# First batch: where the weights' low parts, the range tests and the row flips stand in the order of work

## What is computed

```
attention: state = alpha[t] * state + k[t] (x) v[t];  y[t] = q[t] . state      (alpha in 0.8 to 1.0)
stage 1:   u  = x + Re(FFT over channels (FFT over tokens (x)))
           un = (u - mean) / sqrt(var + 1e-6)
           x2 = u + relu(un @ w_ch1) @ w_ch2          (w_ch1 384x1536, w_ch2 1536x384)
stage 2:   h  = relu(x2^T @ w_tok1) @ w_tok2          (768x256, 256x768)
           u2 = x2 + h^T
           out = u2 + relu(u2 @ w2_ch1) @ w2_ch2
```

## Time and profile before

| what | us |
|---|---|
| median of three runs | 924.83 |
| the profiled execution's own time | 926.65 |
| its span, first to last instruction | 924.9 |
| PE busy | 894.7 (97%) |
| DVE busy | 469.0 (51%) |
| ACT busy | 311.9 (34%) |
| POOL busy | 207.0 (22%) |
| mean granted TensorE clock | 0.990 of full |

### The profile page before, as it was taken

The page is one execution under the profiler, slowest core; times in us unless marked ns, Lnnn a source line. Parts: engine busy times, 40 slices in busy tenths (PEclk is TensorE's granted clock), DMA queues, the critical chain, the costliest instruction groups (busy, mean ns, idle before and its releaser), DMA issues.

```text
span 924.9 us, 14637 instructions
## 1 busy us (share of the span) xinstructions
PE 894.7 (97%) x5376; PEld 861.2 (93%) x5376; DVE 469.0 (51%) x1127; ACT 311.9 (34%) x826; POOL 207.0 (22%) x360
## 2 busy tenths in 40 slices
PE   8978899999999998999999999999999999999998
PEld 5767799998999998999999998999999999999998
DVE  6777876648867658766472216321332142323121
ACT  4663455332555325553323233211121112112111
POOL 3784333302333112333012332000200020002000
PEclk9799999999999999999999999999999999999999
DMA  9803122003030040220017002100200020000000
GB/s 273 323 1 86 31 59 58 27 19 99 26 103 14 27 116 27 59 59 27 1 70 231 26 1 83 46 26 1 76 1 26 0 77 0 26 0 26 0 26 26
DMA packets 14360, 50.81 MB, mean 55 GB/s; under 512 B 1408, under 2 KB 5632, under 8 KB 12368
## 3 DMA queue, kind: packets, MB, share of 16 engines
q1 hardware_dynamic: 13728, 46.95, 16.2%
q0 software_dynamic: 576, 3.15, 0.9%
HBM read 40.66 MB, written 9.44 MB: 54 GB/s over the span
## 4 chain that ended last, share of the span: by engine, by line
PE 87%; DVE 8%; ACT 2%; issue 1%; POOL 1%; DMA 0%; DVEq 0%; ACTq 0%; SPq 0%
PE bank L1141 24%; PE bank L1143 24%; PE bank L1142 24%; PE bank L1155 4%; PE bank L1174 3%; PE bank L1179 2%; PE bank L1164 1%; PE bank L1327 1%; DVE ext L721 1%; PE bank L1321 1%; PE bank L1149 1%; PE bank L1386 1%; PE bank L1274 1%; DVE suf L751 1%; DVE hl L1016 1%
## 5 line engine op out<-in xcount | busy, mean ns | idle before, releaser
L1016 DVE SCALAR_TENSOR_TENSOR hl<-bank,hh 128x384 fp32r<-128x384 f32 x192 | 106.9, 557 | 333.8 <-ACT hh L635 333.7
L635 ACT ACTIVATE hh<-bank 128x384 fp32r<-128x384 f32 x192 | 94.3, 491 | 357.8 <-PE bank L1143 357.8
L1141 PE MATMUL bank<-nh,w1h 128*128 128x384 f32 x288 | 102.6, 356 | 0.5 <-DVE nl L972 0.5
L1141 PE MATMUL bank<-w2h,hh 128*128 128x384 f32 x288 | 101.4, 352 | 0.2 <-DVE u L1031 0.2
L1141 PE MATMUL bank<-u2h,w3h 128*128 128x384 f32 x288 | 97.0, 337 | 0.9 <-DVE u2l L1097 0.9
L1143 PE MATMUL bank<-nh,w1l 128*128 128x384 f32 x288 | 97.5, 339 | 0.0
L1142 PE MATMUL bank<-nl,w1h 128*128 128x384 f32 x288 | 97.2, 337 | 0.0
L1143 PE MATMUL bank<-w2h,hl 128*128 128x384 f32 x288 | 97.0, 337 | 0.0
L1141 PE MATMUL bank<-w4h,hh 128*128 128x384 f32 x288 | 96.9, 337 | 0.0
L1142 PE MATMUL bank<-w2l,hh 128*128 128x384 f32 x288 | 96.6, 335 | 0.0
L1143 PE MATMUL bank<-u2h,w3l 128*128 128x384 f32 x288 | 96.3, 334 | 0.0
(11 more groups left out here) (145 smaller groups left out, 1896.5 us busy)
## 6 DMA issues: line engine op xcount, KB each, us to landing
qkap<-qka SPq DMA_DIRECT2D x15, 1008.0 KB, 6.4
vt<-v SPq DMA_DIRECT2D x16, 288.0 KB, 7.8
raw_a<-w_ch SPq DMA_DIRECT2D x6, 768.0 KB, 10.1
mid<-u SPq DMA_DIRECT2D x8, 576.0 KB, 3.0
raw_b<-w_ch SPq DMA_DIRECT2D x6, 768.0 KB, 5.8
xr<-mid SPq DMA_DIRECT2D x8, 576.0 KB, 4.3
out<-u SPq DMA_DIRECT2D x8, 576.0 KB, 2.8
raw_t<-w_tok SPq DMA_DIRECT2D x2, 768.0 KB, 6.3
```

The lines of the kernel that those rows point to most:

```text
L635: act.activation(hh[:, s % 4, :], bank[s % 2][:, 0:HALF], ACT.Relu).then_inc(s_hhi, 1)
L1016: dve.scalar_tensor_tensor(out=hl[:, s % 4, :], in0=bank[s % 2][:, 0:HALF], scalar=0.0, in1=hh[:, s % 4, :].bitcast(F32), op0=ALU.max, op1 ...
L1141: pe.matmul(out_ap, wh, rh, start=first, stop=False)
```

## The change

- `LOW_AT`, `LATE_LOW_AT`: four half pieces of the low parts are written in visits 12, 14, 16 and 18 of batch 0 (before: eight, in the odd visits from 9); four once the edge rows of batch 0 are copied (before: once x is split); the last four in visits 0, 2, 4 and 6 of batch 1, that is beside MLP 0. PE's wait for all twelve becomes three waits, at MLP steps 2, 6 and 10.
- `RANGE_AT`: the 8 reductions of batch 0 stand one each at the end of visits 1, 2, 5, 7, 9, 11, 13 and 15 (before: in visits 2 and 3, 8 and 9, 10 and 11, 14 and 15).
- `flipped`: the flips of batch 0 go to banks 2 to 4 in place of 5 to 7, `f1` of batch 0 does not wait for their copies, and ACT splits the first half of x before it copies the flips.
- `edge_rows` moves from slot 39 to slot 35, behind the third split of g.
- POOL's v terms of tile 2 wait until the normalised row tile 2 is written (`un_ready`), in every batch.
- `fourier_u` of tiles 4 and 5 moves from slot 45 to slot 46, behind `norm_split` of tile 2, in every batch.
- `fill` gives one spare matmul behind visit 22 and four behind visit 23 (before: none behind either).

```diff
--- before.py
+++ after.py
@@ -36,6 +36,10 @@
 PAUSES = (3, 7, 14, 21, 28)
 WARM = 8
 FILL = {31: 5, 42: 6, 44: 4, 45: 1, 46: 2}
+LOW_AT = (12, 14, 16, 18)
+LATE_LOW_AT = (0, 2, 4, 6)
+RANGE_AT = {1: (1, 0), 2: (1, 1), 5: (2, 0), 7: (2, 1), 9: (0, 0), 11: (3, 0), 13: (3, 1), 15: (0, 1)}
+RANGED = (0, 2, 4, 7)
 VISIT = dict(zip([h for h in range(31) if h not in PAUSES], range(-2, STEPS)))
 SUMS_AT = 31
 F1_AT = 33
@@ -289,6 +293,10 @@
     def turned(a, k):
 
         return visit_bank(a, k - 2)[:, T_AT:T_AT + PR]
+
+    def flipped(a, j):
+
+        return bank[(5 if a else 2) + j][:, 0:DM]
 
     def bad_sum(a):
 
@@ -483,27 +491,29 @@
                 pool.wait_ge(s_rows, a + 1)
                 for j in (1, 2):
                     pool.wait_ge(s_vc, a * 3 + j + 1)
+                    if j == 2:
+                        pool.wait_ge(*un_ready(a, 2))
                     for dst, src, w, op in v_terms(a, j):
                         pool.tensor_tensor(dst, src, w, op).then_inc(s_pv, 1)
 
             pool.wait_ge(s_qk0, 16)
             prep(0, 0)
             tables = ((dfth, dft[0]), (dftl, dft[1]), (csh, cs[0]), (csl, cs[1]))
-            wi = 0
             for k in range(-2, STEPS):
                 visit(0, k)
                 if 3 <= k < 7:
                     pool.dma_start(tables[k - 3][0][:], tables[k - 3][1].bitcast(F32R)).then_inc(s_table, 16)
-                elif k >= 9 and k % 2:
-                    weight_lo(wi)
-                    wi += 1
-            pool.wait_ge(s_xlo, 2 * KT)
-            for i in range(wi, 2 * NA):
+                elif k in LOW_AT:
+                    weight_lo(LOW_AT.index(k))
+            pool.wait_ge(s_rows, 1)
+            for i in range(len(LOW_AT), 2 * NA - len(LATE_LOW_AT)):
                 weight_lo(i)
             for a in range(B):
                 if a:
                     for k in range(-2, STEPS):
                         visit(a, k)
+                        if a == 1 and k in LATE_LOW_AT:
+                            weight_lo(2 * NA - len(LATE_LOW_AT) + LATE_LOW_AT.index(k))
                 fourier_v(a)
                 if a + 1 < B:
                     prep(a + 1, 0)
@@ -569,7 +579,7 @@
                     act.wait_ge(s_mid, MID_PRIMED + 32 * (a - 1))
                 for j in range(3):
                     act.wait_ge(s_flip, a * 3 + j + 1)
-                    act.activation(us[a % 2][:, 2 * j + 1, :], bank[5 + j][:, 0:DM], ACT.Copy).then_inc(s_flipc, 1)
+                    act.activation(us[a % 2][:, 2 * j + 1, :], flipped(a, j), ACT.Copy).then_inc(s_flipc, 1)
 
             def split_x(a, part):
                 act.wait_ge(s_fold, a * 7 + (4, 7)[part])
@@ -615,9 +625,13 @@
 
             def tail(a, h):
                 if h == SUMS_AT:
-                    copy_flipped(a)
-                if h in (SUMS_AT, SUMS_AT + 1):
-                    split_x(a, h - SUMS_AT)
+                    if a:
+                        copy_flipped(a)
+                    split_x(a, 0)
+                if h == SUMS_AT + 1:
+                    if a == 0:
+                        copy_flipped(a)
+                    split_x(a, 1)
                 if 0 <= h - F1_AT < 2 * KT:
                     split_g(a, h - F1_AT)
                 if h in V_AT:
@@ -761,7 +775,7 @@
                 buf, cols = chunk(a, k)
                 decay = buf[0:PR, 2, cols]
                 if k % NC == 0 and (a or k):
-                    dve.wait_ge(s_ext, a * (2 * NU) + 2 * ((k // NC + 1) if a else (3, 1, 2, 4)[k // NC]))
+                    dve.wait_ge(s_ext, a * (2 * NU) + (2 * (k // NC + 1) if a else RANGED[k // NC]))
                 dve.wait_ge(s_inv, a * STEPS + k + 1)
                 dve.tensor_tensor_scan(decay, decay, nothing(a).to_broadcast([PR, P]), inv[0:PR, j:j + 1],
                                        ALU.mult, ALU.add).then_inc(s_pre, 1)
@@ -840,14 +854,14 @@
                     range_flag(a)
                 if 0 <= k + 1 < STEPS:
                     attn_scores(a, k + 1)
-                if k % NC == 3 and 0 <= k and k // NC + 1 < NU:
+                if a and k % NC == 3 and 0 <= k and k // NC + 1 < NU:
                     extreme(a, k // NC + 1, 1)
                 attn_state(a, k + 1)
                 prep(a, k + 3)
-                if k % NC == 2 and k // NC + 1 < NU:
+                if a and k % NC == 2 and k // NC + 1 < NU:
                     extreme(a, k // NC + 1, 0)
-                if a == 0 and k in (10, 11):
-                    extreme(a, 0, k - 10)
+                if a == 0 and k in RANGE_AT:
+                    extreme(a, *RANGE_AT[k])
                 if k + 2 == FLAG:
                     range_test(a)
                 if k in (FLAG + 2, FLAG + 3):
@@ -977,10 +991,10 @@
                     fold(a)
                 if h in (SUMS_AT + 1, SUMS_AT + 2):
                     split_x(a, h - SUMS_AT - 1)
-                if h == F1_AT + 2 * KT:
-                    edge_rows(a)
                 if 0 <= h - F1_AT < 2 * KT:
                     split_g(a, h - F1_AT)
+                if h == F1_AT + 2:
+                    edge_rows(a)
                 if h == 40:
                     fourier_v(a)
                     for i in range(2):
@@ -1003,7 +1017,7 @@
                     norm_rows(a, 2)
                 for t in NORM_AT.get(h, ()):
                     norm_split(a, t)
-                if h == 45:
+                if h == 46:
                     for i in range(2):
                         fourier_u(a, 4, 2, i)
                 if h == SLOTS - 1 and a + 1 < B:
@@ -1215,14 +1229,13 @@
                 if a:
                     pe.wait_ge(s_nlo, a * NC)
                 for j in range(3):
-                    pe.matmul(bank[5 + j][:, 0:DM], flip[:, :], x[:, 5 - j, :], start=True, stop=True
-                              ).then_inc(s_flip, 1)
+                    pe.matmul(flipped(a, j), flip[:, :], x[:, 5 - j, :], start=True, stop=True).then_inc(s_flip, 1)
 
             def f1(a, i):
 
                 part, t = i // KT, i % KT
                 pe.wait_ge(s_xlo, a * 6 + i + 1)
-                if i == 0:
+                if i == 0 and a:
                     pe.wait_ge(s_flipc, a * 3 + 3)
                 if i >= 3:
                     pe.wait_ge(s_glo, a * (2 * KT) + i - 2)
@@ -1329,7 +1342,7 @@
 
             for k in range(-2, STEPS):
                 visit(0, k)
-                fill(1 if 0 <= k < STEPS - 2 else 0)
+                fill(0 if k < 0 else 4 if k == STEPS - 1 else 1)
             pe.wait_ge(s_const2, 32)
             pe.wait_ge(s_table, 64)
             for h in range(SUMS_AT, SLOTS):
@@ -1344,8 +1357,8 @@
                             pe.wait_ge(s_nlo, b * NC + 3 * (s // NF) + 3)
                         mlp_in(b, s, w1h, w1l, nh, nl).then_inc(s_hp, 1)
                     elif s >= 2:
-                        if b == 0 and s == 2:
-                            pe.wait_ge(s_wlo, 2 * NA)
+                        if b == 0 and s in (2, 6, 10):
+                            pe.wait_ge(s_wlo, 2 * (KT + 1 + (s - 2) // FG))
                         mlp_out(b, s - 2, w2h, w2l, s_x2, b * NC + X2_PRIMED)
                     elif b:
                         mlp_out(b - 1, MLP - 2 + s, w2h, w2l, s_x2, (b - 1) * NC + X2_PRIMED)
```

## The result

The changed kernel takes 929.19 us (median of 13 runs, 926.63 to 937.58), the kernel before on the same chip 924.86 (13 runs, 924.09 to 928.88): ratio 1.0049, 95% interval 1.0029 to 1.007. That is 4.3 us slower, and 3.9 above the forecast of 925.3, inside its range. The profiled execution took 932.0 us, with a span of 930.2.

The account below looks back on a forecast made before the run. PE bounds the kernel, busy 97% of the span, with most idle time in batch 0's first 108 us. Terms sum to +0.5 on the profiled 926.65, giving 927.15; less 1.8 for the median, 925.3 us, range 919.5 to 930.0.

Parts of the forecast that it names:

- the collision: After `f1` in batch 0, POOL's later pieces hold up DVE's four v additions, delaying PE: 3.7 us, plus 0.9 of half clock.
- the two losses: POOL's later pieces holding DVE's additions (3.7 us, 0.9 for half clock) and `fourier_u` delaying PE at batch ends (2.9).
- The second rival: Half clock stays in the visits, so the 3.0 us isn't gained: 929.6 us, chance 0.2.
- Clock in the visits: Batch 0's visits: evenly spaced reductions remove the half clock from 36.8 to 47.0 us; gain 3.0, bounds 0 and 5.1.
- the range test is free: In batch 0's visits, POOL's pieces no longer hold DVE's range test: 0.7 us gained.
- Low parts in the visits: Batch 0's visits: four POOL pieces instead of eight delay products less; gain 1.3 us, bounds 0 and 3.8.
- Range tests: Batch 0's visits: one pair of reductions and six single ones cost DVE 4.1 us, not 5.3; gain 1.2.
- Sums, flips, split: Batch 0 after the visits: undisturbed sums and full-clock flips let `f1` begin 5.6 us behind the sums, not 7.7; gain 2.1.
- spare matmuls: The one behind visit 22 delays visit 23's output, costing 0.3 us; four behind visit 23 fill PE's wait and keep clock.
- Four later pieces: Behind `f1` in batch 0, pieces waiting for edge rows delay DVE's additions and PE's second u product: 3.7 us lost.
- the half clock behind the stall: After PE idles 4.7 us in batch 0, spare matmuls run at half clock in half of executions: 0.9 us lost.
- `fourier_u`: At three batch ends, running it behind the last split makes PE wait longer: 2.9 us lost, bounds 0 and 3.1.

Follow-up runs that it names:

- a3: Changed kernel with POOL's four later pieces waiting for the split of x again and `fourier_u` of tiles 4 and 5 back in slot 45: 920.91 us, ratio 0.9933.
- a1: Changed kernel with one edit undone: POOL's four later pieces wait for the split of x again, not the edge rows; 924.72 us, ratio 0.9984.
- a2: Changed kernel with one edit undone: `fourier_u` of tiles 4 and 5 back in slot 45; 925.79 us, ratio 0.9998.
- a4: a3 with ACT's first high part of a weight in visit 8 instead of 6: 919.34 us, ratio 0.9926.
- c3: a4 without the line that holds back POOL's v terms of tile 2: 918.96 us, ratio 0.9933.
- b3: Kernel before with only the new places of the range reductions, at most one a visit: 921.52 us, ratio 0.9961.
- a6: a4 with POOL's four pieces in visits 10, 12, 14 and 18 instead of 12, 14, 16 and 18: 918.32 us, ratio 0.9924.
- b1: Kernel before with only `fourier_u` of tiles 4 and 5 moved to slot 46: 929.24 us, ratio 1.0046.
- c1: Kernel before with only the changed tail of batch 0 (flips' banks, `f1` without a wait, ACT's split first, spare matmuls): 925.59 us, ratio 0.9997.
- c2: Kernel before with only the low parts' new places and PE's three waits, four pieces still waiting for the split of x: 923.15 us, ratio 0.9976.
- b2: Kernel before with only the edge rows copied earlier, behind the split of g, and POOL's four later pieces waiting for them: 931.99 us, ratio 1.0069.

## Why the prediction was right, and where it failed

**The number** was 3.9 us low. The mechanism that I called likeliest (gains in the visits and before `f1`, eaten by the collision and the batch ends) is there in all its pieces. By the times, the two losses were sized too small: 10.7 us between after and a3, where my terms have 7.5. The gains were about right: without the losses my terms leave 7.0, and a3 is 6.2 under the kernel before (4.5 to 7.8). 3.2 and 0.8 make up the 3.9 but for a tenth. The second rival, the half clock that stays in the visits, comes to 929.6 by its working, next to the measured 929.19, but that is luck: by it a3 would be 7.5 lower, 922.1 and 2.7 under the kernel before, which is outside a3's interval.

**Clock in the visits (-3.0).** In the profiles of after's own code this gain isn't there: 10.2 and 3.4 us of half clock in after, 6.8 in a1, 3.4 in a2, 10.2 in a3, 6.8 in a4, none in c3, against 10.2 in before. The cause that I had named, the pairs of reductions, is borne out by the thirteen profiles, and with the range tests alone (b3) the visits kept 1.00 and the time fell by 3.6 us. What I had wrong is that nothing would take the place of the pairs. In after it was two stops of PE, 2.10 for `qz` behind ACT's late weight load and 1.70 for the flag; in the other kernels with after's visits it was the second alone. So the step that failed is the sentence that the range test is free, in the next term. How the times of a3 hold most of the gain all the same isn't settled by one profile of each. The mean clock of every execution is on record, though, and by it a3's six have 10 us of half clock each over the whole span (an estimate, twice the missing clock times the span) and the kernel before on the same chip 18.5; some of that is the 3.4 us in the flips, which no profile with after's tail has.

**Low parts in the visits (-1.3).** The places alone are worth 2.2 us, forecast 2.5 with the late sum, but by another sum than mine: I wrote that the range test is free now (0.7). It isn't, and this is the mechanism that I had wrong. Before, the piece of visit 15 held L779 for 1.51 us and PE waited 0.31 for the flag; the piece of visit 16 holds L795 for 2.22 and PE waits 1.70. All six profiles with a piece in visit 16 beside after's range tests show it, a6 without one doesn't. With the clock at 1.00 in both, the late sums of a6 start 1.1 us ahead of c3's (62.05 and 63.18): about so much the piece's place in visit 16 costs without a fall of the clock. My lower bound for this term was wrong too: four new pieces at the full 1.8 would cost 7.2, against the 3.8 and 0.7 that they replace, a loss of 2.7 and not 0.

**Range tests (-1.2).** Compared at like clocks the late sums start 1.3 us (b1 to a1, 0.93), 2.3 (before to a3, 0.90) and 3.3 earlier (c1 to c3, 1.00, where c3's high parts are later too); my terms for range tests and pieces give 2.5.

**Sums, flips, split (-2.1), spare matmuls (+0.3).** The leg came out right in the profile: the sums undisturbed, the flips at full clock, `f1` 5.18 us behind the sums (5.6 forecast), 2.5 gained and the spare matmul behind visit 22 not seen in the last visit. But c2 shows that the pieces' new places do it alone: with the old order of the tail its late sums take 0.83, its flips 2.17 at full clock, and `f1` follows 4.70 behind the sums. Its flips begin 0.72 behind them and after's 1.27, since there the four spare matmuls stand ahead: they cost about 0.5 here, and what they were to keep, the clock, c2 kept without them. The part alone (c1) gave 0.3 in the times, as its share of the terms, though its profile shows `f1` 6.10 behind the sums and not 7.72. There the stretch behind 100 us ran at a clock of 0.68 (0.83 before), and MLP to end was 827.1 (825.95): some of the gain was given back at the start of the MLP.

**Four later pieces (+3.7) and the half clock behind the stall (+0.9).** Place and order were right: the pieces began 5.20 us behind `f1` (5.25 forecast), the additions 9.77 (9.8), all four were held. Sizes were off both ways: the stall is 2.94 (3.94 - 1.00), the half clock 1.5 (4.46 of the leg less 2.94). I had three additions follow the fourth piece; the second was over 0.2 us behind it (88.09 and 87.88), and the last two took 1.27 together, so that all ended 13.9 behind the start of `f1`. I had written 14.7, where my own steps (12.5 for the pieces, 0.3, three times 0.5) add up to 14.3. The Trainium skill ("SBUF — State Buffer", "Who interferes with whom"), by whose rule I had 2.7, was nearer than my 3.7. In the times the part costs more than in the profile of after, 6.0 to 6.4 us; b2's profile shows where it can go (28.25 - 22.15 = 6.1, with the longer half clock). The two terms together were undersized by 1.4 to 1.8.

**`fourier_u` (+2.9).** Right by the trace: 0.92 at the first batch end (1.66 - 0.74), 0.93 at each other, 2.8 in all. The times say 4.2 to 4.7, with 2.9 just outside b1's interval (3.0 to 5.5); what makes up the rest isn't shown. From the MLP to the end the edit adds 2.3 and 2.4 us where profiles can be paired (a2 825.96 and after 828.21, before 825.95 and b1 828.36), and 4.8 from a3 (826.60) to a1 (831.44); of these 4.8, 1.6 lie behind 558, where a1 alone had half clock again (0.66 from 560 to 565).

**Four pieces beside MLP 0 (+0.3) and the held v terms (0).** Nothing seen against either; c3 bears out the second (0.9933, a4 0.9926, with 1.4 and 1.8 us to either side).

**What stays open.** Which stop of PE is followed by the half clock: c3 had the same 1.70 us for the flag as a1 and a3, and kept 1.00. Why b2 and c2 had one behind the flag at waits of 0.31 and 0.95, and before, b1 and c1 none at 0.31. And why a6, undisturbed through the visits, is hardly faster in the times than a4: like c3, it had 6.8 us of half clock later, at the start of the MLP, and a4 3.4.

## What to carry to other kernels

When work is moved off a busy stage, look for what it stands beside next: here a piece of 1.8 us on POOL stopped DVE's additions in one place and a 0.46 us test in another, and each stop reached PE. A wait that is moved onto a later event (here one small copy) must be timed against whoever uses the other side of the shared resource afterwards; 0.5 us of margin was enough, 2.7 us too late cost 6. A clock term needs a look at what else stops PE in the same stage: with one cause gone (the pairs), the clock fell behind the next (the flag). And one profile is too few for it: of six with the same stop, five fell.

## What was unexpected of the hardware

- A tiny DVE instruction can be passed over twice: L795 began at 54.31, 0.01 us behind POOL's L475, and did not end when that did (54.76) but when the next POOL instruction, begun at 54.71, had ended (56.51). The additions at 85.15 and 86.14 took turns with the pieces instead.
- DVE's reductions never stretched: L735 took 920 to 948 ns in all 32, the one at 46.57 beside a piece that ran from 45.95 to 47.76 among them.
- The first load into `raw_a` in after took 20.9 us from its issue at 7.63 to the issue at 28.54 that waits for its landing; in the twelve other profiles that was 15.7 to 19.4 (23.29 in a6, 27.04 in c2). The slowest of the six took 25.3, in the others 17.3 to 24.1. In ACT's in-order list the first one alone stopped PE for 2.10 us, once.
